# Normalising spread over two phases, split inner rows, and M1 ahead of M4 in a fused attention and MoE kernel

## The reference

```python
def reference_core(q, k, v, ...):
    # 1: retention attention, B=4, H=8, S=576, D=64
    ret = (scale * q @ k.T) * Dmat          # Dmat: gamma**(i-j), causal
    x = (ret @ v), heads joined             # 2304 tokens x 512
    # 2: gated layer, d_ff = 1536
    xn = x / sqrt(mean(x*x) + 1e-6) * rms_g
    g = xn @ w_gate
    x = (g * sigmoid(g) * (xn @ w_val)) @ w_out
    # 3: top-1 mixture of 8 experts, 512 -> 1024 -> 512, with an output gate
    ...
```

## Time and profile before

| | |
|---|---|
| median of 3 runs | 882.36 us (881.67 to 883.47) |
| the profiled execution | 893.08 us, of which the span is 891.1 us |
| PE busy | 803.2 us (90% of the span) |
| DVE, ACT, POOL busy | 519.7, 425.7, 450.9 us |
| DMA, mean | 112 GB/s |
| mean granted TensorE clock | 0.964 |
| chain that ended last | PE 70%, POOL 10%, DVE 9%, issue 5%, ACT 3% |

### The profile page before, as it was taken

How to read it: one execution, slowest core, us unless ns; L and a number is a source line. 1 busy time by engine, 2 the same in 40 slices (tenths; PEclk the granted TensorE clock), 3 DMA queues, 4 the chain that set the end, 5 groups by cost and what they waited for, 6 DMA issues and landing times.

```text
span 891.1 us, 14837 instructions
## 1 busy us (share of the span) xinstructions
PE 803.2 (90%) x5053; PEld 706.5 (79%) x5053; DVE 519.7 (58%) x798; ACT 425.7 (48%) x815; POOL 450.9 (51%) x384
## 2 busy tenths in 40 slices
PE   7997688877899999789999999972999999999995
PEld 6886578776679999667999978842888888888884
DVE  3577678998535888653688632351455454554553
ACT  3564464444445555354655423521355454455453
POOL 3568976667754888664688523156112112222221
PEclk9998899999999999799999999987999999999998
DMA  9982012113121223212124012311545545556553
GB/s 317 318 285 86 24 49 70 48 48 95 48 60 36 72 88 125 76 55 60 29 76 143 28 47 67 123 37 32 172 144 163 185 155 169 177 160 173 161 169 103
DMA packets 48362, 99.65 MB, mean 112 GB/s; under 512 B 7490, under 2 KB 8644, under 8 KB 48295
## 3 DMA queue, kind: packets, MB, share of 16 engines
q1 hardware_dynamic: 42934, 87.40, 31.1%
q0 software_dynamic: 4944, 10.96, 4.2%
q10 hardware_dynamic: 432, 0.63, 0.2%
HBM read 89.50 MB, written 10.40 MB: 112 GB/s over the span
## 4 chain that ended last, share of the span: by engine, by line
PE 70%; POOL 10%; DVE 9%; issue 5%; ACT 3%; another core or an unknown queue 2%; DMA 1%; SPq 0%; POOLq 0%; ACTq 0%; DVEq 0%
PE banks L1392 7%; PE banks L1394 6%; PE banks L1393 6%; PE banks L1446 5%; PE banks L1579 5%; PE banks L1580 5%; PE banks L1448 5%; PE banks L1447 5%; PE banks L1581 5%; PE banks L1379 4%; PE banks L1380 4%; PE banks L1381 4%; POOL AL L493 3%; POOL AL L487 2%
## 5 line engine op out<-in xcount | busy, mean ns | idle before, releaser
L1392 PE MATMUL banks<-BH,AH 128*128 128x384 f32 x504 | 175.4, 348 | 29.7 <-DVE g L779 13.3
L1393 PE MATMUL banks<-BL,AH 128*128 128x384 f32 x504 | 171.2, 340 | 0.0
L1394 PE MATMUL banks<-BH,AL 128*128 128x384 f32 x504 | 171.1, 339 | 0.0
L1392 PEld LDWEIGHTS banks<-BH,AH 128*128 128x128 f32 x504 | 96.0, 191 | 41.5 <-DVE g L779 16.5
L809 DVE TENSOR_TENSOR hidL<-hid,hidH 128x384 fp32r<-128x384 f32 x72 | 55.8, 780 | 91.9 <-ACT hidH L1086 91.9
L493 POOL TENSOR_TENSOR AL<-s_ab,AH 128x1024 fp32r<-128x1024 f32 x36 | 94.7, 2631 | 12.5 <-ACT AH L1064 12.3
L1446 PE MATMUL banks<-dH,hidH 128*128 128x512 f32 x216 | 87.4, 405 | 12.9 <-DVE hidL L809 12.9
L1394 PEld LDWEIGHTS banks<-BH,AL 128*128 128x128 f32 x504 | 96.4, 191 | 0.0
L1393 PEld LDWEIGHTS banks<-BL,AH 128*128 128x128 f32 x504 | 96.2, 191 | 0.0
L505 POOL TENSOR_TENSOR dL<-wraw,dH 128x512 fp32r<-128x512 f32 x36 | 49.0, 1362 | 85.6 <-ACT dH L1079 85.6
L1579 PE MATMUL banks<-wH,h2H 128*112 128x512 f32 x192 | 77.7, 405 | 14.4 <-DVE h2L L963 14.4
(11 more groups left out here) (179 smaller groups left out, 1723.2 us busy)
## 6 DMA issues: line engine op xcount, KB each, us to landing
wraw<-w_moe SPq DMA_DIRECT2D x168, 256.0 KB, 2.7
wraw<-w_moe SPq DMA_DIRECT2D x36, 512.0 KB, 3.6
vr<-v_rows SPq DMA_DIRECT2D x15, 320.0 KB, 4.6
qt<-q_t SPq DMA_DIRECT2D x16, 288.0 KB, 4.6
y_rows<-y_sb SPq DMA_DIRECT2D x6, 768.0 KB, 6.0
kt<-k_t SPq DMA_DIRECT2D x15, 288.0 KB, 4.3
kr<-k_rows SPq DMA_DIRECT2D x16, 256.0 KB, 3.2
mask<-c_mask SPq DMA_DIRECT2D x4, 160.0 KB, 5.5
```

The lines of the kernel that those rows point to most:

```text
L1392: mm(to, wh, bh, start=first and k == 0, stop=False, skip_group_check=True)
L1393: mm(to, wh, bl, start=False, stop=False, skip_group_check=True)
L1394: i = mm(to, wl, bh, start=False, stop=k == 1, skip_group_check=True)
```

## The change

- `root` and `normalise` for batches 2 and 3 get buffers of their own (`late`, beside `hid`), so they need not wait for older ones. In the up phase of block 0 each group f = 0 to 10 gets one piece (3 root steps of batch 2, 8 calls of `normalise`, `IN_UP`), always behind hid1; 11 more (`IN_DOWN`) go into the down phase. None is left at the end of attention for batch 2.
- PE's order: M1 of the next group stands ahead of M4 of this one; M3 of the next follows M4. DVE takes g0 of the next group (`first_gate`) ahead of hid0.
- The last group of every block: the two halves of the first down step stand between M6 and M7 and between M7 and M4. For that `high_hidden`, `low_hidden`, `high_down` and `low_down` of step 0 come one group earlier.
- Entry of the layer: `norm(2)` comes one unit later on PE, `sums_a` of the first two groups goes from POOL to DVE (`sums_four`), so do the low halves of T3 and NT4 of block 0 (`low_first`), POOL's and ACT's work is put in another order, batch 3's `mean_square` comes ahead of the first sigmoid, and a block's products start M2, M1, M5, M3.
- ACT takes the last three banks of a block one by one in the next block's first groups (`take_y`). Token sums, `high_b` and `low_b` are spread differently over the down steps.
- SP: the two first loads of down weights (256 KB each) leave attention for group 2 of block 0.

```diff
         h_stack = ExitStack()
         hid = sb_in(h_stack, "hid", [P, F1, BLOCK])
+        late = sb_in(h_stack, "late", [P, 4, SEQ])
...
-            return SCORES + 1 if b == BATCH - 1 else out_bank((b + 1) * PAIRS) + 1
+            return (out_bank(PAIRS) + 1, out_bank(2 * PAIRS) + 1, out_bank(3 * PAIRS + 1) + 1, SCORES + 1)[b]
 
...
+        def statistics(b):
+
+            return (late[:, 3, :], late[:, 2, :]) if b == BATCH - 1 else (ms[:, b % 2, :], r0[:, b % 2, :])
+
+        def inverse(b):
+
+            return rinv[:, b, :] if b < 2 else late[:, b - 2, :]
+
         def x_part(blk, b):
...
+        def lows(blk, b):
+
+            return blk * 7 - (len(DVE_LOW) if blk > 0 else 0) + b + 1
+
+        DOWN_B = {0: B21, 1: B11, 2: B22, 3: T1, 5: T2, 6: T3, 7: NT4}
         N_KV, N_QK = 2 * 16, 2 * 16
         UNITS = BATCH * PAIRS
...
-                if u in (10, 12):
-                    f = (u - 10) // 2
-                    sp.dma_start(wraw[:, f, UPC:W1COLS], plane(w_moe1, f)[:, UPC:W1COLS]).then_inc(s_wd[f], 16)
...
                     weights1_up(n0 + f + 4)
+                    if blk == 0 and f == 2:
+                        for p in range(2):
+                            sp.dma_start(wraw[:, p, UPC:W1COLS], plane(w_moe1, p)[:, UPC:W1COLS]).then_inc(s_wd[p], 16)
...
                     add_squares(u - 1)
+                if u == 9:
+                    low_a(0)
                 if u == 10:
-                    sums_a(0)
                     low_b(0, B21)
                 if u == 11:
                     low_b(0, B11)
-                    low_a(0)
                 if u == 12:
                     low_S(0)
                 if u == 13:
+                    low_b(0, B22)
+                if u == 14:
+                    low_b(0, T1)
+                if u == 15:
                     low_b22(0)
-                if u == 14:
-                    low_b(0, B22)
-                    sums_a(1)
-                    low_a(1)
-                if u == 15:
-                    low_b(0, T1)
             low_b(0, T2)
+            low_a(1)
             low_S(1)
-            low_b(0, T3)
             low_b22(1)
-            low_b(0, NT4)
             for blk in range(BLOCKS):
                 n0 = blk * F1
                 for f in range(F1):
+                    if f >= F1 - 2:
+                        low_down(n0 + f - F1 + 2)
                     sums_a(n0 + f + 2)
                     low_a(n0 + f + 2)
                     low_S(n0 + f + 2)
                     low_b22(n0 + f + 2)
-                    if f >= F1 - 2:
-                        low_down(n0 + f - F1 + 2)
                 for f in range(F1):
                     if f < F1 - 2:
                         low_down(n0 + f + 2)
-                    if blk + 1 < BLOCKS and f < 7:
-                        low_b(blk + 1, f)
+                    if blk + 1 < BLOCKS and f in DOWN_B:
+                        low_b(blk + 1, DOWN_B[f])
...
+
+            def sums_four(n):
+
+                sums_two(n)
+                r = wraw[:, n % 2, :]
+                dve.wait_ge(s_Sd, 4 * n + 1)
+                V.tensor_tensor(s_ab[:, 1, :], s_ab[:, 0, :], r[:, 0:HK], ALU.subtract).then_inc(s_Sd, 1)
+                dve.wait_ge(s_Sd, 4 * n + 3)
+                V.tensor_tensor(s_ab[:, 3, :], r[:, HK:2 * HK], s_ab[:, 1, :], ALU.subtract).then_inc(s_Sd, 1)
...
+            def low_first(b):
+
+                dve.wait_ge(s_BH, b + 1)
+                V.tensor_tensor(BL[:, b], t3[:] if b == T3 else x_part(0, b), BH[:, b].bitcast(F32),
+                                ALU.subtract).then_inc(s_BLd, 1)
...
                 if u == 9:
-                    sums_two(0)
+                    sums_four(0)
                 if u == 13:
-                    sums_two(1)
                     sums_b(0, T3)
                     sums_b(0, T1)
                 if u == 14:
-                    root(2, HALVE, TIMES)
-                    normalise(2, 0)
+                    sums_b(0, T2)
                 if u == 15:
-                    sums_b(0, T2)
                     sums_b(0, NT4)
-                    root(2, FIX)
+                    sums_four(1)
 
             decay_scores(0)
...
+            def first_gate(n):
+
...
+            def hidden(n, between=(), then=(), last=()):
+
+                x, f = banks[:, X[n % 2]:X[n % 2] + 1, 0:HALF], n % F1
+                if f == 0:
+                    first_gate(n)
                 sums_two(n + 2)
                 dve.wait_ge(s_m6, n + 1)
...
@@ -788,19 +827,20 @@
                 dve.wait_ge(s_sig1, n + 1)
                 wait(dve, s_h1, n)
                 V.tensor_tensor(hv[:, 1:2, :], g1[:], sig[:, 1:2, :], ALU.mult).then_inc(s_hv1, 1)
+                run(between)
                 dve.wait_ge(s_m7, n + 1)
...
                 dve.wait_ge(s_hv1, n + 1)
                 V.tensor_tensor(hid[:, f:f + 1, HALF:BLOCK], hv[:, 1:2, :], v1[:], ALU.mult).then_inc(s_h1, 1)
-                for task in more[0:1]:
-                    task()
+                run(then)
+                if f < F1 - 1:
+                    first_gate(n + 1)
                 dve.wait_ge(s_m4, n + 1)
                 dve.wait_ge(s_hv0, n + 1)
                 V.tensor_tensor(hid[:, f:f + 1, 0:HALF], hv[:, 0:1, :], x, ALU.mult).then_inc(s_h0, 1)
-                for task in more[1:]:
-                    task()
+                run(last)
 
             def low_hidden(m):
...
-            LATER = ([norm_task(2, k) for k in range(1, KD)] + [norm_task(3, k) for k in range(KD)] + [root_task(3, i) for i in range(3)]
-                     + [norm_task(4, k) for k in range(KD)] + [norm_task(5, k) for k in range(KD)])
+            def low_task(m):
+                return lambda: low_hidden(m)
+
+            IN_UP = [root_task(2, i) for i in range(3)] + [norm_task(q, k) for q in (2, 3) for k in range(KD)]
+            IN_DOWN = [root_task(3, i) for i in range(3)] + [norm_task(q, k) for q in (4, 5) for k in range(KD)]
+            DOWN_T = {0: T3, 1: T1, 4: T2, 6: NT4}
             for blk in range(BLOCKS):
                 n0 = blk * F1
                 for f in range(F1):
-                    hidden(n0 + f, LATER[2 * f:2 * f + 2] if blk == 0 else ())
-                low_hidden(2 * n0)
-                low_hidden(2 * n0 + 1)
+                    hidden(n0 + f, [low_task(2 * n0 + 1)] if f == F1 - 1 else (), IN_UP[f:f + 1] if blk == 0 else (),
+                           [low_task(2 * n0)] if f == F1 - 2 else ())
                 for f in range(F1):
-                    if blk + 1 < BLOCKS and f == 0:
-                        sums_b(blk + 1, T3)
-                        sums_b(blk + 1, T1)
-                    if blk + 1 < BLOCKS and f == 4:
-                        sums_b(blk + 1, T2)
-                        sums_b(blk + 1, NT4)
                     if f < F1 - 1:
                         low_hidden(2 * (n0 + f + 1))
+                    if blk + 1 < BLOCKS and f in DOWN_T:
+                        sums_b(blk + 1, DOWN_T[f])
+                    if f < F1 - 1:
                         low_hidden(2 * (n0 + f + 1) + 1)
+                    if blk == 0:
+                        run(IN_DOWN[f:f + 1])
 
 
...
+                if u == 3 * PAIRS + 1:
+                    act.wait_ge(s_norm, 3)
...
+                if b < BATCH - 1:
+                    wait(act, s_rinv, (b - 1) * 3)
+                m, r = statistics(b)
...
+                    if n < 2:
+                        act.wait_ge(s_Sd, 4 * (n + 1))
+                    else:
+                        act.wait_ge(s_S, 2 * (n - 1))
...
-                    S.activation(y_sb[:, (2 * blk + a) * TPH + j, :], banks[:, DOWN[a][j], :], ACT.Copy).then_inc(s_y, 1)
+                S.activation(y_sb[:, (2 * blk + a) * TPH + j, :], banks[:, DOWN[a][j], :], ACT.Copy).then_inc(s_y, 1)
...
+                blk, f = n // F1, n % F1
...
-                if n == 0:
-                    high_b(0, NT4)
...
-                if n == 1:
-                    mean_square(BATCH - 1)
-                if n % F1 >= F1 - 2:
-                    high_down(n - F1 + 2)
+                if blk > 0 and f < TPH:
+                    take_y(blk - 1, 1, f)
+                if f == F1 - 3:
+                    high_down(n - f)
+                if f == F1 - 2:
+                    high_hidden(2 * (n - f))
+                    high_hidden(2 * (n - f) + 1)
+                    high_down(n - f + 1)
 
             def down_step(n, blk):
 
                 f = n % F1
                 if f < F1 - 1:
                     high_hidden(2 * (n + 1))
-                    high_hidden(2 * (n + 1) + 1)
                 if f < F1 - 2:
                     high_down(n + 2)
-                if blk + 1 < BLOCKS and f < 7:
-                    high_b(blk + 1, f)
+                if f < F1 - 1:
+                    high_hidden(2 * (n + 1) + 1)
+                if blk + 1 < BLOCKS and f in DOWN_B:
+                    high_b(blk + 1, DOWN_B[f])
...
-                if u in (5, 9, 13):
```

(74 more changed lines are left out.)

72 lines of the change are left out of this document (34 added, 38 removed).

## The result

The changed kernel takes 877.86 us (median of 8 runs, 872.76 to 880.52), the kernel before beside it 883.54 (8 runs, 881.60 to 886.45): a ratio of 0.992, 95% interval 0.989 to 0.994. Faster, by 0.8%, where 3.2% was predicted; 877.86 lies 10 us above the upper end of the range.

What follows compares the result with a forecast made beforehand. PE was the engine to watch; in block 0 it waited for g0, with DVE setting the pace. Terms -9.9 - 15.2 - 2.3 + 1.5 - 2.9 - 0.5 + 1.1 = -28.2 us took 882.36 to 854.2 us; range 844 to 861.

Steps and rivals of the forecast that it cites:

- Down phase of block 0: Block 0's 11 down steps: eleven pieces cause two more waits for `hidL`, +1.5 us; bounds 0 and +9.
- the parts on blocks 1 and 2: Blocks 1 and 2: M1 ahead of M4 0, up-phase ends -2.9 and -0.5, starts +1.1 us.
- Entry: Attention and layer entry, to g0 of group 1: stall at `norm(2)` goes and g0 comes earlier, -9.9 us.
- ends at about 83: End of attention: its last product comes at about 83 in place of 88.3 us.
- ACT's chain: Entry: last square, NT4, `high_S(1)`, mean square and `copy_m5` on ACT lie under the DVE and POOL queue.
- The forecast for group 0: Block 0's first group, behind the entry: 8.4 us in place of 8.8.
- The sum of 15 us for the shared queue: Entry: DVE's 5.5 and POOL's 10 us of SBUF work exclude each other, both ending 15 us after 80.5.
- Ten groups of block 0: Block 0's up phase: hid1 gets in ahead of `low_S`, beat 8.25 us, ten groups 82.9 against 98.06, -15.2 us.
- Blocks 1 and 2, up phase: Regular groups of blocks 1 and 2: M1 ahead of M4 changes nothing, 0 us, hidden by 0.47 us of idle.
- the fourth rival: All three blocks: late sums make hid1 miss `low_S`, long beat everywhere, +10 us, 892; chance 0.06.
- Ends of the up phases: Last group and step 0: down halves fill waits but bring their own; -2.3, -2.9, -0.5 us in blocks 0, 1, 2.
- Carried over unchanged: Whole kernel: the profiled execution's saving of 28.2 us applies unchanged to the median of 882.36 us.

Runs made afterwards that it cites:

- a_down_order: Changed kernel with one edit: in a down step ACT splits both hidden halves first and the down weight last, as before the change; 871.0 us, ratio 0.976.

## Why the prediction was wrong, by its steps

**Down phases: the step that failed.** The part "Down phase of block 0" costed what DVE got there, the pieces, and the parts on blocks 1 and 2 had no term for the down phase at all. The diff moves one more instruction in `down_step`, `high_down(n + 2)` on ACT, and the prediction didn't walk it through. The down phases were 17.3 of the 21 us. The rule that it had at hand, whoever is in first holds the other out for a whole instruction, was applied to hid1 and not to `hidL`; both directions of the edit show that it decides there too (-15.3 us, +22.6 us). The 3.5 us that stay open are those named with `a_down_order`. The bound of +9 stood for the pieces in block 0, so the range missed the same loss three times over. The pieces themselves cost 0 in place of 1.5 (50.50 against 50.46).

**Entry: -5.0 in place of -9.9.** The sentence that the last product of attention "ends at about 83" failed: the layer's first product stayed at 88.20, since the sums moved to DVE made a wait of 3.25 us in unit 10. The prediction took them off POOL's queue and put nothing for them on DVE's inside attention. It also let "ACT's chain" lie under the queue, where M3 of group 0 waited 2.83 us for it. With them on POOL it is 84.05, and g0 of group 0 92.88, where 92.5 was forecast. The forecast for group 0, 8.4 us, was too short as well: 9.42 measured, 10.3 with the earlier start, as g1 stands behind `low_S(1)`. (The sum of 15 us for the shared queue gives 95.5 from 80.5; that g0 would come at 92.5, ahead of its end, was judged and not added up.)

**Ten groups of block 0: right.** -13.7 against -15.2; beat 8.15 to 8.17 in seven of the ten, against 8.25. Group 1, still behind the entry's queue, took 9.92, and the group ahead of the last 8.93, which the forecast didn't have. The mechanism (early g0 puts hid1 ahead of `low_S`) is shown by the run that takes it away (9.45) and the one that adds it to the kernel before (8.8 with two pieces). The forecast split the piece's price into 0.5 us by which it ends behind `low_S` and 0.37 net for the operations around it; the run with narrow pieces shows 0.36 for the width, which is what ends behind `low_S`, and 0.44 for the rest. The forecast, 82.9 us for the ten, lies between the two executions (84.38, 82.70).

**Blocks 1 and 2, up phase: right.** g0 to g0 stays at 7.3 to 7.4 us in the regular groups; nothing of the fourth rival shows. By the rule of the Trainium skill (SBUF — State Buffer, Who interferes with whom) which of the two engines issues first decides who is held up. The rows here agree: 0.94 for hid1 ahead of `low_S` and 2.72 behind it, 0.56 for `hidL` ahead of `low_down` and 1.33 behind it. Who is first was decided in the down steps by the order of issue on a third engine, ACT. M3 directly behind M5 waits 0.58 us (0.75 forecast), and M5 ahead of M1 gives back 0.85.

**Ends of the up phases: right in kind, low in size.** -2.0, -3.8 and -3.1 against -2.3, -2.9 and -0.5. Three waits were foreseen, 0.9 us for `hidL` of half 0 and 1.7 each for half 1 and for step 1. Block 1 has none, 2.06 and 1.82; block 0 has 0.53, none and 1.82, and 0.97 for g0, which was not foreseen. The -3.8 of block 1 are partly luck, as its clock stayed at 1.00; with 12.57 us it is -2.3. In block 2 the forecast (-0.5) took the waits there for too short to win from: the run without the interleaving loses 3.8 us from g0 of group 10 on.

**The profile's own time.** "Carried over unchanged" was harmless here, but 8.6 of the 15.8 us between the two profiled executions lie in a layer that is the same code: a profile must be compared by its stages, not by its span.

## What to carry to other kernels

Walk every moved instruction through, on every engine, also where that engine is busy 40% of the time: between two engines that exclude each other, an instruction of 0.6 us moved on a third one decides which of them is in first, once in every step. A stall that goes because work was moved to another queue has to be looked for again in that queue, at what stands behind the work there. And when a phase ends later after a change, look at the waits of its plainest repetition (here block 2) before suspecting what was added in the busiest.

## What the runs showed of the hardware

A DVE operation on 16 columns, both inputs in SBUF, took 2.37 us behind a POOL operation of 2.58 that had started 0.25 us before it, and one on 384 columns in the same place 2.75: how long it was shut out did not depend on its own size. The same waits (2.06 and 2.08 us, then 1.82 and 1.81) were followed by a granted clock of 1.00 in one execution and 0.86 in another, 1.5 us apart. The kernel before differs by 1% between chips, and the layer of routed experts, by the same code, took 312.2 us in one job (152 GB/s moved) and 325.0 in another (146 GB/s), with PE busy 293.0 and 294.6 us. What lies behind it was not tried.
